# Placing row numbers and gates in bf16, and one block for a route and its expert layer

## The chip, the cores and the metric

The kernel runs on one core of one Trainium2 chip. The time is the device time of one execution in microseconds; what is compared is the median of several runs. Besides there is a profile of one execution.

## The reference

An attention layer with decaying state, then two mixture-of-experts layers, all over 3072 rows of 384 numbers (4 sequences of 768 steps, 8 heads of 48).

```
cur = u*k_t (x) v_t;  y_t = r_t (state + cur);  state = w*state + k_t (x) v_t
layer 1: rows with x.w_skip > 0:  e = argmax(x w_gate), g = softmax(x w_gate)[e]
         out = x + g * relu(x w1[e]) w2[e];  other rows: out = x
layer 2: the same for all rows, without the added x:  out = g * relu(x w1b[e]) w2b[e]
```

There are 8 experts of 384 x 1024 and 1024 x 384. Each row goes to one of them.

## The kernel before

`network` runs `attention`, then twice `route` and `moe`. The order on each engine is written out by hand, with semaphores between engines; `attention`, each `route` and each `moe` is a block of its own (`nc.Block()`), and at the end of a block every engine drains and waits for the others.

`route` makes a table. The 3072 rows lie as 24 tiles of 128: row r of tile i on partition r. For each row the route finds its expert, its rank among that expert's rows, and from them a place (`slot_i`) in a list in which each expert's rows begin at a tile of their own. The table has 128 partitions and NCOL columns (38 in the first layer, 45 in the second); column c holds the places of tile c: word 0 is the number of the row of x that stands there, word 1 its gate. Places that stay empty hold a number beyond the rows (NOWHERE), which the gathers skip.

Rows are put in their places by products. For tile i, `row_hot[:, i, :]` (128 x 128) is one where the row's place modulo 128 is the column, and `placing` (128 x 2 x NCOL) holds at the column of the row's place the row number and the gate. Their product, summed over the 24 tiles in one bank (`ps_placed`), is the table. All is f32. VectorE makes the column one-hots (L687), the gates' words (L690) and the row one-hots (L541, 8 of 3 tiles each); ScalarE makes the row numbers' words (L632, 24 small ones); TensorE multiplies (L617, which the profile shows as 48 records) after it has been kept busy by `stay_warm` (L22, 64 transposes of the identity). VectorE then writes `starts` (the spans of tiles of each expert) and the table (L709, L710).

Between these, ScalarE and VectorE split the first expert's weights in two fp32r parts (L763 `W.hi`: rounded; L768 `W.lo`: the residue). There are 6 pieces of w1 and 8 of w2. In the first route three of VectorE's pieces come before the table.

`moe` begins with a head: GpSimd gathers the first X row tiles by the table (L1006; X is 2 in the first layer, 4 in the second); TensorE loads its spans into registers, turns the identity (L1096 and 24 turns by `stay_warm`), then turns each gathered tile (L1090); ScalarE rounds it (L1244), VectorE takes the residue (L1314). Then comes a loop over the experts and, within one, over units of 192 or 256 rows (first layer) or 384 or 448 (second). In a unit the products to the hidden numbers go in 8 groups of 9 (L1107 to L1109: hi x hi, hi x lo, lo x hi for each of 3 chunks) through 4 banks; from the fifth group on TensorE waits for VectorE's residue of the hidden numbers (L1354) four groups before. VectorE makes pieces of the next weights between. The products back (`ps_y`) are scaled by the gate (L1331) and scattered by GpSimd. SyncE loads the weights.

## Time and profile before

| | |
|---|---|
| median of 3 runs | 570.91 us (569.67 to 571.74) |
| the profiled execution | 574.45 us, of which the span is 572.7 us |
| attention | until 133.6 us |
| first route, table written | 133.6 to 151.0 us |
| first layer's head, first expert product | 151.0 to 159.9 us |
| second route, table written | 310.8 to 328.1 us |
| second layer's head, first expert product | 328.1 to 338.1 us |
| TensorE busy | 94% of the span |

The span is what the trace covers; the execution's own time has 1.8 us around it. Engines: PE is TensorE, PEld its weight loads, DVE VectorE, ACT ScalarE, POOL GpSimd, SP SyncE; PEq and so on are their sequencers. A line such as L617 is that of the kernel. PEclk is the granted share of TensorE's clock of 2.4 GHz, 0.5 being its lower level of 1.2 GHz.

### The profile page before, as it was taken

To read this page: it belongs to the slowest core of one execution; us is meant where nothing else is said; L and a number is where in the kernel's file an instruction comes from. 1 tells how busy PE (TensorE), PEld (TensorE's weight loads), DVE (VectorE), ACT (ScalarE), POOL (GpSimd) and SP (SyncE) were. 2 spreads that over 40 slices of the span, in tenths; PEclk is the share of its full clock that TensorE was granted. 3 is DMA by queue.
4 is the path that set the end of the run, shared out by engine and by line. 5 is a ranking of instruction groups with operands and counts; after the bars stand their busy time and mean duration, and the time that the engine had idled before them with its cause. 6 is when DMAs were issued, how large, how long until landed. Compare 5 with 4: busy or idle time off the path is not lost. (4 is left out here: it accounts for less than half of the span.)

```text
span 572.7 us, 16167 instructions
## 1 busy us (share of the span) xinstructions
PE 537.0 (94%) x5557; PEld 510.8 (89%) x5558; DVE 381.7 (67%) x839; ACT 264.4 (46%) x758; POOL 247.4 (43%) x357
## 2 busy tenths in 40 slices
PE   4899999997889999999988879999999999999994
PEld 4789998986889999999976869999999999999994
DVE  4788888876788878888845727473747464737331
ACT  0233333333567656777733326362736352627230
POOL 5887778752144554444412061322433323324241
PEclk9999999997899999999999989999999999999998
DMA  8788889858177876774568523444444544111101
GB/s 154 127 178 166 161 163 175 166 203 286 31 251 255 256 232 195 227 256 130 159 197 284 177 81 132 162 149 151 165 155 150 169 138 155 51 43 46 42 1 40
DMA packets 114130, 89.60 MB, mean 156 GB/s; under 512 B 80672, under 2 KB 104931, under 8 KB 114080
## 3 DMA queue, kind: packets, MB, share of 16 engines
q1 hardware_dynamic: 105744, 73.96, 45.8%
q0 software_dynamic: 7776, 14.82, 9.4%
q8 instruction: 26, 0.43, 0.3%
q10 hardware_dynamic: 560, 0.20, 0.2%
q14 instruction: 24, 0.20, 0.1%
HBM read 80.44 MB, written 13.27 MB: 164 GB/s over the span
## 5 line engine op out<-in xcount | busy, mean ns | idle before, releaser
L768 DVE TENSOR_TENSOR w_lo<-w_raw,w_hi 128x384 fp32r<-128x384 f32 (+1 forms) x224 | 129.9, 606 | 5.4 <-ACT w_hi L763 3.4
L1107 PE MATMUL e_ps_h<-e_x_hi,w_hi 128*128 128x192 f32 (+3 forms) x384 | 119.9, 312 | 2.7 <-DVE e_x_lo L1314 2.7
L763 ACT CAST w_hi<-w_raw 128x384 fp32r<-128x384 f32 (+1 forms) x224 | 120.1, 566 | 4.4 <-issue 4.4
L1109 PE MATMUL e_ps_h<-e_x_hi,w_lo 128*128 128x192 f32 (+3 forms) x384 | 119.7, 312 | 0.5 <-issue 0.5
L1108 PE MATMUL e_ps_h<-e_x_lo,w_hi 128*128 128x192 f32 (+3 forms) x384 | 119.8, 312 | 0.0
L1354 DVE SCALAR_TENSOR_TENSOR e_h_lo<-e_ps_h,e_h_hi 128x128 fp32r<-128x128 f32 (+1 forms) x192 | 70.3, 395 | 45.2 <-ACT e_h_hi L1262 41.1
L1107 PE MATMUL e_ps_y<-w_hi,e_h_hi 128*128 128x384 f32 x272 | 95.6, 351 | 0.0
L1109 PE MATMUL e_ps_y<-w_hi,e_h_lo 128*128 128x384 f32 x272 | 91.4, 336 | 0.0
L1108 PE MATMUL e_ps_y<-w_lo,e_h_hi 128*128 128x384 f32 x272 | 91.3, 336 | 0.0
L1107 PEld LDWEIGHTS e_ps_h<-e_x_hi,w_hi 128*128 128x128 f32 x384 | 73.2, 191 | 5.1 <-DVE e_x_lo L1314 3.2
L1109 PEld LDWEIGHTS e_ps_h<-e_x_hi,w_lo 128*128 128x128 f32 x384 | 73.1, 190 | 0.9
L1108 PEld LDWEIGHTS e_ps_h<-e_x_lo,w_hi 128*128 128x128 f32 x384 | 73.1, 190 | 0.9
L1261 ACT ACTIVATE e_h_lo<-e_ps_h 128x64 fp32r<-128x64 f32 x128 | 29.2, 228 | 76.8 <-PE e_ps_h L1109 69.2
L1262 ACT ACTIVATE e_h_hi<-e_ps_h 128x256 fp32r<-128x256 f32 (+1 forms) x128 | 59.6, 465 | 0.0
L1314 DVE TENSOR_TENSOR e_x_lo<-e_ps_x,e_x_hi 128x384 fp32r<-128x384 f32 (+1 forms) x54 | 28.1, 523 | 43.9 <-ACT e_x_hi L1244 37.5
L1108 PEld LDWEIGHTS e_ps_y<-w_lo,e_h_hi 128*128 128x128 f32 x272 | 51.3, 188 | 0.0
L1107 PEld LDWEIGHTS e_ps_y<-w_hi,e_h_hi 128*128 128x128 f32 x272 | 51.2, 188 | 0.0
L1109 PEld LDWEIGHTS e_ps_y<-w_hi,e_h_lo 128*128 128x128 f32 x272 | 51.1, 188 | 0.0
L1244 ACT CAST e_x_hi<-e_ps_x 128x384 fp32r<-128x384 f32 (+1 forms) x54 | 24.4, 455 | 54.5 <-PE e_ps_x L1090 54.5
L1015 POOL DMA_INDIRECT x_in<-x_rows,e_ent_in x33 | 37.1, 1125 | 26.8 <-POOL e_ent_in L1011 22.0
L1027 POOL DMA_INDIRECT out_dram<-y_rows,e_ent_out x19 | 18.5, 974 | 62.5 <-DVE y_rows L1331 54.3
L224 ACT COPY xT<-ps_x 128x384 f32<-128x384 f32 x24 | 11.5, 480 | 71.0 <-PE ps_x L368 71.0
(192 smaller groups left out, 928.8 us busy)
## 6 DMA issues: line engine op xcount, KB each, us to landing
w_raw<-in_moe_w_dram SPq DMA_DIRECT2D x32, 1536.0 KB
r_in<-in_r_dram SPq DMA_DIRECT2D x24, 192.0 KB, 3.1
k_in<-in_k_dram SPq DMA_DIRECT2D x24, 192.0 KB, 3.9
v_in<-in_v_dram SPq DMA_DIRECT2D x24, 192.0 KB, 3.9
x_rows<-rows SPq DMA_DIRECT2D x24, 192.0 KB, 3.5
w_raw<-x_rows SPq DMA_DIRECT2D x4, 768.0 KB, 7.8
e_late_x<-x_rows SPq DMA_DIRECT2D x2, 768.0 KB, 6.1
x_in<-x_rows,e_ent_in POOLq DMA_INDIRECT x33, 3.0
```

What stands on the lines that cost most here:

```text
L763: act.copy(self._of(self.hi1[par], self.hi2[par], n), self._of(self.raw1[par], self.raw2[par], n)).then_inc(self.hi_done[par], 1)
L768: eng.tensor_tensor(self._of(self.lo1[par], self.lo2[par], n), self._of(self.raw1[par], self.raw2[par], n), self._of(self.hi1[par], self.h ...
L1015: pool.indirect_dma_start(x_in[n][:], None, rows, bass.IndirectOffsetOnAxis(ap=ent_in[n][:, 0:1], axis=0), bounds_check=bound, oob_is_err= ...
L1027: pool.indirect_dma_start(out_rows, bass.IndirectOffsetOnAxis(ap=ent_out[slot][0:count, 0:1], axis=0), y_rows[slot][0:count, :], None, bou ...
L1107: pe.matmul(o, s_hi, m_hi, start=(k == 0), stop=False)
L1108: pe.matmul(o, s_hi, m_lo, start=False, stop=False)
L1109: return pe.matmul(o, s_lo, m_hi, start=False, stop=(k == last))
L1244: act.copy(x_hi[:, :, w], ps_x[n % 2][:, 0:D].rearrange("p (c t) -> p c t", c=DC)[:, :, 0:w.stop - w.start]).then_inc(x_hi_done, 1)
L1261: act.activation(h_lo[:, k, top_at:top_at + HALF], ps_h[k % 4][:, TOP], ACT.Relu).then_inc(h_top_done, 1)
L1262: act.activation(h_hi[:, k, :], ps_h[k % 4][:, 0:XW], ACT.Relu).then_inc(h_hi_done, 1)
L1314: dve.tensor_tensor(x_lo[:, :, w], ps_x[n % 2][:, 0:D].rearrange("p (c t) -> p c t", c=DC)[:, :, 0:w.stop - w.start], x_hi[:, :, w].bitcas ...
L1354: ins = dve.scalar_tensor_tensor(h_lo[:, k, lo_at[n]:lo_at[n] + of.stop - of.start], ps_h[k % 4][:, of], 0.0, h_hi[:, k, of].bitcast(F32), ...
```

## The change

1. A route and its layer are in one block. In place of the block's end, semaphores (`routed`, `gates_split`, `gates_placed`) hold back what needs the table.
2. Layouts are turned: `row_hot` is [128, 128 columns, 24 tiles] and `col_is` [128, NCOL, 24], with the tile as the inner dimension, in bf16. They come from 16-bit integers: `at` (row and column of each place) and one large `iota` [128, 128, 24] that GpSimd makes once. The column one-hots are one instruction, the row one-hots three (8 tiles each).
3. The row number is placed as two bf16 words that are added afterwards: `tile_word` (128 x the tile's number, less NOWHERE, which is now 4096; VectorE multiplies) and `own_word` (the partition; ScalarE multiplies). A first product of `ones` and `empty` adds NOWHERE to every place. The products read `row_hot[:, :, i]` and `id_words[:, :, :, i]`.
4. Gates leave the route. GpSimd splits them in three bf16 pieces; VectorE spreads these over the columns right behind the table (two instructions), and TensorE places them in the layer's head, 12 tiles before the first gathered tile is turned and 12 after it, into `ps_y[1]`; VectorE adds the three and writes word 1 of the table. `stay_warm` there has 1 turn of 8 in place of 3.
5. VectorE's first pieces of w1 go from the route to the head: all 6 before the first `x_low`, all 8 of w2 after the gates.
6. GpSimd copies only word 0 of the table for its gathers and scatters. The layer's tiles stand in another order in memory.

```
-            for n in range(PLACES):
-                if n % (PLACES // 2) == 0:
-                    pe.wait_ge(gates_placed, 2 * n // PLACES + 1)
-                pe.wait_ge(ids_placed, n + 1)
+            pe.wait_ge(words_made, 4)
+            pe.matmul(ps_ids, ones[:], empty[:], start=True, stop=False)
+            pe.wait_ge(tile_words, 1)
+            pe.wait_ge(own_words, 1)
+            for n, part in enumerate(PARTS):
                 pe.wait_ge(rows_ready, n + 1)
-                for q in range(GP):
-                    i = GP * n + q
-                    ins = pe.matmul(ps_placed, row_hot[:, i, :], placing[:, 2 * NCOL * i:2 * NCOL * (i + 1)], start=(i == 0), stop=(i == TILES - 1))
-                ins.then_inc(placed, 1)
+                for i in range(part.start, part.stop):
+                    ins = pe.matmul(ps_ids, row_hot[:, :, i], id_words[:, :, :, i], start=False, stop=(i == TILES - 1))
+            ins.then_inc(placed, 1)
...
-            for place in range(PLACES):
-                if place % (PLACES // 2) == 0:
-                    act.wait_ge(col_equal, 2 * place // PLACES + 1)
-                for i in range(GP * place, GP * place + GP):
-                    ins = act.mul(col_hot[:, i, 0, :], col_is[:, i, :], entry[:, i, 0:1])
-                ins.then_inc(ids_placed, 1)
+            act.mul(id_words[:, 1, :, :].rearrange("p c i -> p (c i)"), col_is[:].rearrange("p c i -> p (c i)"), own_word[:, 0:1]).then_inc(own_words, 1)
...
-            for n in range(2):
-                i = slice(TILES // 2 * n, TILES // 2 * (n + 1))
-                wide = [P, TILES // 2, NCOL]
-                dve.tensor_tensor(col_is[:, i, :], row_iota[:, 0:NCOL].unsqueeze(1).to_broadcast(wide),
-                                  col_i[:, i].unsqueeze(2).to_broadcast(wide), ALU.is_equal).then_inc(col_equal, 1)
-                dve.wait_ge(col_equal, n + 1)
-                dve.tensor_tensor(col_hot[:, i, 1, :], col_is[:, i, :], entry[:, i, 1].unsqueeze(2).to_broadcast(wide), ALU.mult).then_inc(gates_placed, 1)
-                for place in range(PLACES // 2 * n, PLACES // 2 * (n + 1)):
-                    rows_hot(dve, place)
-            if m == 0:
-                for n in range(W.N1 // 2):
-                    W.lo(dve, 0, 0, n)
+            dve.tensor_tensor(col_is[:], iota[:, 0:NCOL, :], at[:, 1, :].unsqueeze(1).to_broadcast([P, NCOL, TILES]), ALU.is_equal).then_inc(col_equal, 1)
+            link(dve.tensor_scalar(at[:, 0, :], slot_i[:], P - 1, None, ALU.bitwise_and))
+            dve.tensor_tensor(id_words[:, 0, :, :], col_is[:], tile_word[:].unsqueeze(1).to_broadcast([P, NCOL, TILES]), ALU.mult).then_inc(tile_words, 1)
+            for part in PARTS:
+                dve.tensor_tensor(row_hot[:, :, part], iota[:, :, part], at[:, 0, part].unsqueeze(1).to_broadcast([P, P, part.stop - part.start]), ALU.is_equal).then_inc(rows_ready, 1)
...
-            dve.wait_ge(placed, PLACES)
-            dve.tensor_scalar(table[:, 0:NCOL, 0], ps_table[:, 0, :], float(NOWHERE), None, ALU.add)
-            dve.tensor_copy(table[:, 0:NCOL, 1].bitcast(F32), ps_table[:, 1, :])
+            dve.wait_ge(placed, 1)
+            link(dve.tensor_reduce(ids[:], ps_ids.rearrange("p w c -> p c w"), AX.X, ALU.add))
+            dve.tensor_copy(table[:, 0:NCOL, 0], ids[:]).then_inc(routed, 1)
...
+            pe.wait_ge(routed, 1)
             start_spans(pe)
...
-            stay_warm(pe, ident, ps_y[0][:, 0:P], 3)
-            for n in range(X):
+            stay_warm(pe, ident, ps_y[0][:, 0:P], 1)
+            for n, some in enumerate(HALVES):
+                pe.wait_ge(gates_spread, n + 1)
+                for i in range(some.start, some.stop):
+                    ins = pe.matmul(ps_gates, row_hot[:, :, i], gate_words[:, :, :, i], start=(i == 0), stop=(i == TILES - 1))
+                if n == 0:
+                    turn_x(0, 0)
+            ins.then_inc(gates_placed, 1)
+            for n in range(1, X):
                 turn_x(0, n)
...
-            dve.sem_inc(y_done, 1)
+            dve.wait_ge(gates_split, 5)
+            for some in HALVES:
+                wide = [P, 3, NCOL, some.stop - some.start]
+                dve.tensor_tensor(gate_words[:, :, :, some], col_is[:, :, some].unsqueeze(1).to_broadcast(wide), pieces[:, :, some].unsqueeze(2).to_broadcast(wide), ALU.mult).then_inc(gates_spread, 1)
+            dve.wait_ge(routed, 1)
             start_spans(dve)
...
             if m == 0:
-                for n in range(W.N1 // 2, W.N1 + 2):
+                for n in range(W.N1):
                     W.lo(dve, 0, 0, n)
             for n in range(X):
                 x_low(0, n)
-            if m == 0:
-                for n in range(W.N1 + 2, W.N):
+            dve.wait_ge(gates_placed, 1)
+            dve.tensor_reduce(table[:, 0:NCOL, 1].bitcast(F32), ps_gates.rearrange("p w c -> p c w"), AX.X, ALU.add).then_inc(y_done, 1)
+            if m == 0:
+                for n in range(W.N1, W.N):
                     W.lo(dve, 0, 0, n)
...
+            with ExitStack() as both:
+                block = both.enter_context(nc.Block())
+                late = route(nc, both, block, m, W, ...)
+                moe(nc, both, block, m, W, ..., *late)
```

## Rows read from the trace of the kernel before

**Rows 1.** The page: TensorE's line, and its clock by slice.

```profile
PE 537.0 (94%) x5557; PEld 510.8 (89%) x5558; DVE 381.7 (67%) x839; ACT 264.4 (46%) x758; POOL 247.4 (43%) x357
...
PEclk9999999997899999999999989999999999999998
```

**Rows 2.** Timeline, first route: start, us taken, engine, line, operation.

```profile
136.66 8.65 PE L22 MATMUL m_ps_spare<-ident 128*128 128x128 f32 x64
...
141.64 0.63 DVE L687 TENSOR_TENSOR m_col_is<-m_row_iota,m_col_i 128x456 f32<-128x456 int32 x1
...
142.86 1.96 DVE L541 TENSOR_TENSOR m_row_hot<-m_row_iota,m_row_i 128x384 f32<-128x384 int32 x4
...
145.15 5.48 PE L617 MATMUL m_ps_places<-m_placing,m_row_hot 128*128 128x76 f32 x48
...
148.02 3.39 ACT L763 CAST w_hi<-w_raw 128x384 fp32r<-128x384 f32 x8
...
150.78 0.19 DVE L710 COPY table<-m_ps_places 128x38 f32<-128x38 f32 x1
```

**Rows 3.** Timeline, head of the first layer and first expert.

```profile
152.63 1.21 POOL L1006 DMA_INDIRECT rows<-x_rows,table  x1 [15.83 <-issue]
...
152.88 0.63 PE L1096 MATMUL e_ps_h<-ident 128*128 128x128 f32 x4 [2.24 <-issue]
...
153.34 4.45 PE L22 MATMUL e_ps_y<-ident 128*128 128x128 f32 x24
...
154.14 1.54 POOL L1006 DMA_INDIRECT x_in<-x_rows,table  x1 [0.30 <-issue]
...
157.96 0.49 PE L1090 MATMUL e_ps_x<-ident,x_in 128*128 128x128 f32 x3
...
159.60 2.91 DVE L768 TENSOR_TENSOR w_lo<-w_raw,w_hi 128x384 fp32r<-128x384 f32 x6
...
159.94 0.35 PE L1107 MATMUL e_ps_h<-e_x_hi,w_hi 128*128 128x192 f32 x1 [1.50 <-DVE e_x_lo L1314]
...
161.03 0.28 PE L1107 MATMUL e_ps_h<-e_x_hi,w_hi 128*128 128x192 f32 x1
...
162.44 0.48 DVE L1354 SCALAR_TENSOR_TENSOR e_h_lo<-e_ps_h,e_h_hi 128x128 fp32r<-128x128 f32 x2
```

**Rows 4.** Timeline, second route and head of its layer.

```profile
313.20 0.50 PE L606 MATMUL m_ps_places<-m_chosen,m_ones 128*128 128x192 bf16 x1 [1.13 <-DVE m_chosen L659]
313.52 0.27 PE L607 MATMUL m_ps_places<-m_chosen,m_neg_lower 128*128 128x192 bf16 x1
...
322.28 5.49 PE L617 MATMUL m_ps_places<-m_placing,m_row_hot 128*128 128x90 f32 x48
...
327.93 0.20 DVE L710 COPY table<-m_ps_places 128x45 f32<-128x45 f32 x1
...
329.26 1.10 POOL L1006 DMA_INDIRECT rows<-x_rows,table  x1 [12.99 <-issue]
...
333.28 1.00 POOL L1006 DMA_INDIRECT x_in<-x_rows,table  x1 [0.30 <-issue]
...
336.36 0.55 PE L1090 MATMUL e_ps_x<-ident,x_in 128*128 128x128 f32 x3 [0.79 <-DMA x_in<-x_rows,table]
...
338.14 0.68 PE L1107 MATMUL e_ps_h<-e_x_hi,w_hi 128*128 128x384 f32 x1 [1.24 <-DVE e_x_lo L1314]
```

**Rows 5.** Lines 606, 607: ns min/median/max, first and last start, shapes.

```profile
L606 PE MATMUL m_ps_places<-m_chosen,m_ones x2: 500/502/503, 136.2 to 313.2; 128*128 128x192 bf16 x2
...
L607 PE MATMUL m_ps_places<-m_chosen,m_neg_lower x2: 266/302/337, 136.5 to 313.5; 128*128 128x192 bf16 x2
```

**Rows 6.** Line 677, the same columns.

```profile
L677 DVE TENSOR_TENSOR m_pos<-m_ps_places,m_seen x2: 612/614/617, 139.2 to 316.3; 128x192 f32<-128x192 f32 x2
```

**Rows 7.** Line 1002, GpSimd's first instruction in the layer's block.

```profile
L1002 POOLq MOVE  x2: 29/29/29, 151.6 to 328.4; - x2
```

**Rows 8.** Window 338 to 342 us; chain of waits there.

```profile
338.00:342.00 4.00, 3.86 (x14) 3.86 (x15) 0.00 (x0) 0.63 (x3) 2.47 (x4) 0.61 0.22 60
...
338.83 0.32 PE e_ps_h L1108
...
341.50 0.17 PE e_ps_h L1108
```

## What I expect of the change

> **What bounds the kernel now.** I read the page first: TensorE is busy 94% of the span [rows 1], so time can be won or lost only where TensorE does work that is not the expert products, or waits. The slices of the page show where: its granted clock dips between 129 and 157 us and again from 329 us (tenth, eleventh and 24th slice of 14.3 us) [rows 1]; together with the names of the lines this leads to two places, the two routes with the head of the expert layer behind each. I then read the timeline of each, since a share of busy time hides order there.
>
> Route of the first layer [rows 2]: TensorE turns the identity 64 times until 145.31 us, only to keep warm. VectorE starts the column one-hots at 141.64 us, and the placing products run from 145.15 to 150.63 us: 48 records in 5.48 us, 0.114 us each, 24 products of two passes. So TensorE sets the end here, as the first product starts when the warming ends. The table is written by 150.97 us. The route of the second layer has the same form: 5.49 us of placing from 322.28 us, the table at 328.13 us [rows 4].
>
> Head of the first layer [rows 3]: GpSimd's first gather starts at 152.63 us, 1.66 us behind the table; the second row tile is turned at 157.96 us and the first expert product starts at 159.94 us, 8.97 us behind the table. Between them lie 4.45 us of warming, which end at 157.79 us. Head of the second: table 328.13, first gather 329.26, fourth gather 333.28, its turn 336.36 (3.08 us later), first product 338.14 us: 10.01 us [rows 4]. The gathers, 1.34 us apart, set that one.
>
> **What the change does with each, in a sum.** Times are given behind the table (R) where that is shorter.
>
> *The row numbers.* The 24 products in f32 (48 records) become 24 in bf16 plus one short one that fills in the empty places. Both operands are now read with a step: tiles are the inner dimension of the one-hots and of the words, so neighbouring weight columns and neighbouring moving columns are 24 elements, 48 bytes, apart. No row shows that exactly. The nearest is the product of L606, whose moving operand is read 16 bytes apart: 0.50 us for 192 columns in both instances, beside 0.27 to 0.34 us for L607, whose operand has no step [rows 5]. Some 0.08 us of the 0.50 is that it comes first after a wait and 0.19 us is what every record carries beyond its columns (L607 at full clock: 0.27 less 192 columns at 2.4 GHz, 0.08). That leaves about 0.24 us, 1.25 ns a column, where the operand without step has 0.42. Taken whole, 0.32 us from L606's start to L607's [rows 4] is 1.67 ns. VectorE's L677, which reads 96 bytes apart, has 0.61 us for 192 elements, where 384 without a step take 0.55 [rows 2, 6]; less some 0.13 us fixed that is 2.5 ns an element, the worst row there is. The weights have 128 columns, more than the 76 or 90 that move, and weight loads overlap with products (in the first expert 192 columns take no longer than the load: 0.11 us a product), so the pace is that of the load: 0.06 to 0.10 us if the step costs the load nothing (0.10 is the record of a bf16 load), 128 x 1.25 = 0.16, 128 x 1.67 = 0.21, or 128 x 2.5 = 0.32 us. I take 0.16, from the nearest row, and keep both ends. 24 x 0.16 plus 0.1 for the short product is 3.95 us, so the products end at 149.1 in place of 150.63, and at 326.2 in place of 327.77: **-1.5 and -1.55 us**.
>
> VectorE must be ahead of that. It makes 912 + 912 + 3 x 1024 elements in five instructions where it made 4 x 456 + 8 x 384 in twelve: the same 4896. By the four of L541 in 1.96 us, 0.47 us for 384 [rows 2], an instruction costs 1.04 ns an element and 0.07 us. From 141.45 us that makes the three parts of the row one-hots ready at about 144.95, 146.1 and 147.3 us; TensorE wants them at 145.15, 146.5 and 147.8. Nothing is late, even if the 16-bit types bring no speed at all. ScalarE's word of 912 elements replaces 24 small products and lies under VectorE. GpSimd's large iota (3072 elements) comes before 139 us, and its five small instructions that split the gates wait for nothing that is wanted soon. Hidden, all of it: VectorE first needs them behind the table.
>
> *The table.* One reduction and a copy that waits for it replace two independent copies. By L710 (0.19 us) that is 0.5 us against 0.34: **+0.15 us, twice, +0.3**.
>
> *The block between route and layer.* All engines now go on at a semaphore. In the first layer the block ended at 151.6 us, when ScalarE was done with its 8 casts at 151.41 [rows 2, 7]; in the second at 328.4 [rows 7], 0.25 us behind the table. GpSimd then still needs about 1.0 us before its first gather (151.6 to 152.63). So the gather starts at R + 1.1 in both, against 1.66 and 1.13: 0.5 us in the first layer and nothing in the second. Whether it counts depends on TensorE.
>
> *The gates, now in the head.* 2 x 12 products stand in TensorE's queue between the warming (8 turns in place of 24) and the turns of the row tiles. TensorE: register loads until R + 1.1 (152.88 less 151.6, and the semaphore), 12 turns of the identity until 2.5. The moving operand has 114 and 135 columns; the pace by the same rate is 0.16 and 0.17 us. First layer: first half until 4.4, tile 0 (landed at 1.1 + 3.1 = 4.2) until 4.85, second half until 6.8, then tile 1 (landed at 5.7), and from there 1.98 us to the first product as before (157.96 to 159.94): 8.8 against 8.97, **-0.2 us**. Second layer: halves end at 4.55 and 7.05, tiles 1 and 2 by 7.95; tile 3 waits until the residue of tile 1 is taken out of its bank, 8.8 (its gather landed at 8.2); plus 1.78 us to the product: 10.55 against 10.01, **+0.5 us**. VectorE: two gate products of 1.5 us each at one element a cycle, then six residues of w1 at 0.6 us (three stood in the route before, under TensorE's products), free at 6.7, before tile 1's cast at about 7.4. Hidden.
>
> *Behind the head of the first layer.* VectorE had 6 residues of w2 left before the first hidden residue, from 159.60 us to 162.44, and that one was done 3.0 us after the first product [rows 3]; now it has the reduction of the gates (about 0.3 us) and 8, so it comes some 1.3 us later. TensorE wants it for its fifth group; a group of nine products takes 1.09 us at first (159.94 to 161.03 us) [rows 3] and 1.0 after, so 4.0 us after its start; it will come at some 4.4: **+0.45 us**, and VectorE has no slack to give it back for the rest of this product.
>
> *The clock.* In the second head TensorE is nearly idle from the end of the warming to 338.14 us, and the granted clock of 338 to 342 is 0.61 [rows 8]: the first ten or so products take 0.32 us where they take 0.17 a little later, 1.5 us lost. With the gates' products there it is busy until R + 7 and idle for stretches under a microsecond after that. I expect full clock at the first product: **-1.5 us**.
>
> The sum is -1.5 - 1.55 + 0.3 - 0.2 + 0.5 + 0.45 - 1.5 = **-3.5 us**. The profiled execution, 574.45 us with 572.7 of span, would have 571; it is 3.5 above the median of the runs shown, 570.91, so the median goes to **567.4 us**. A measurement here tells 0.3% (1.7 us) from nothing.
>
> On the operands' step the Trainium skill (Advanced Engine Details and Errata, Memory Cachelines) speaks against the change: accesses that each hit another 16-byte line of SBUF pay a penalty. L606 agrees as far as a row can [rows 5]. It gives no price; with the penalty of L606 on both operands my sum is what stands above, without it -5 us.
>
> **Rivals.** *The step costs TensorE nothing on loads and little on columns* (pace 0.10 or less). Then VectorE sets the routes: 147.3 + 0.8 = 148.1 (-2.6) and 325.5 (-2.2), the head of the first layer is set by VectorE's queue (free at 6.7, two residues, product at 8.0: -1.0), the second stays at the gathers (0), with +0.3 and +0.45: -5.05 us; if VectorE is twice as fast on 16-bit operands, up to -6.5: **564.4 to 565.9 us**. For it: all records of weight loads in the trace have no step, so only the moving side is shown to pay. Chance 0.27. The Trainium skill (VectorE: DVE Perf Modes, The perf-mode tier table) has `tensor_tensor` at 2x when all is 16-bit; no row shows it, and it counts only in this case, for the last 1.4 us.
>
> *The load with a step is dear.* Place: the 24 weight loads of each of the four placements. Each 0.01 us more on the pace costs 24 x 0.01 x 4 = 0.96 us. The gain is gone at a pace of 0.196 us, and it is slower by over 0.3% from 0.214, which is L606's upper reading. At 0.213: -3.5 + 5.1 = +1.6, **572.5 us**; at VectorE's 2.5 ns, +11.9, **582.8 us**. Loads that do not overlap (0.16 + 0.10) come to the same side. For it: 48 bytes are further apart than L606's 16, and both operands step at once. Against it: L606's moving operand paid only 1.25 ns. Chance 0.20.
>
> *Nothing measurable*: pace 0.18 to 0.21, or 0.16 with the clock still falling in the second head (+1.5) and at half in the first as well (there it is full at 159.94 because of the long warming that is cut; another 1.5): -0.5 us, **569.2 to 572.6 us**. Chance 0.15. The forecast itself, pace 0.12 to 0.18, has 0.38, with its own range of 565.5 to 569.2.
>
> So faster 0.65, same 0.15, slower 0.20. The range goes from 563.8 (the fast end, a little more) to 573.2, which leaves out most of the dear loads.
>
> **What would show it.** In the trace after: the interval of the row-number products in both routes (0.16 us; 0.10 or 0.21 decide the rivals); the row one-hots 1.2 us each, or 0.6; R to the first gather 1.1 us; the first expert product at R + 8.8 and R + 10.5; its interval in the second layer 0.17 us at once; a wait of about 0.4 us on VectorE before the fifth group of the first expert. The prediction is wrong if the interval is not near 0.16, if the gates end later than tile 1's landing by more than I have, or if fetching the code after the removed block end costs time that the trace does not show now.

## The result, and the profile after

The change makes the kernel slower. Its median is 575.93 us (575.41 to 577.75, 4 runs), that of the kernel before 570.5 us on the same chip (569.67 to 571.74, 4 runs): a ratio of 1.0099, interval 1.0068 to 1.013. I had predicted 567.4 us, and the value lies above my range. The profiled execution took 577.75 us, with a span of 576.0; before it was 574.45 and 572.7.

The page's clock by slice shows the two places again. Both dips are longer than before [rows 1], and the second reaches a 5.

```profile
PE 543.3 (94%) x5527; PEld 512.8 (89%) x5528; DVE 381.3 (66%) x831; ACT 255.9 (44%) x712; POOL 255.5 (44%) x372
...
PEclk9999999997789999999998859999999999999998
```

The timeline of the first route and head of the changed kernel (start, us taken, engine, line, operation) is to be read against [rows 2, 3]:

```profile
134.00 3.12 POOL L576 IOTA iota<- 128x3072 int16 x1
...
135.30 1.86 DVE L665 TENSOR_SCALAR m_den<-m_den 128x24 f32<-128x24 f32 x1
...
141.59 0.63 DVE L687 TENSOR_TENSOR m_col_is<-iota,m_at 128x912 bf16<-128x912 int16 x1
...
143.74 3.54 PE L623 MATMUL m_ps_ids<-m_id_words,m_row_hot 128*128 128x76 bf16 x24 [0.78 <-DVE m_row_hot L693]
...
147.66 0.19 DVE L709 CAST table<-m_ids 128x38 int32<-128x38 f32 x1
...
148.14 1.56 POOL L1014 DMA_INDIRECT rows<-x_rows,table  x1 [8.01 <-DVE table L709]
...
148.97 1.08 PE L1105 MATMUL e_ps_h<-ident 128*128 128x128 f32 x4 [1.69 <-issue]
...
151.55 2.63 PE L1110 MATMUL e_ps_y<-m_gate_words,m_row_hot 128*128 128x114 bf16 x12
...
154.35 2.61 PE L1110 MATMUL e_ps_y<-m_gate_words,m_row_hot 128*128 128x114 bf16 x12
...
158.76 0.53 PE L1123 MATMUL e_ps_h<-e_x_hi,w_hi 128*128 128x192 f32 x1 [1.16 <-DVE e_x_lo L1335]
...
322.64 4.09 PE L623 MATMUL m_ps_ids<-m_id_words,m_row_hot 128*128 128x90 bf16 x24
...
327.12 0.19 DVE L709 CAST table<-m_ids 128x45 int32<-128x45 f32 x1
...
330.84 3.08 PE L1110 MATMUL e_ps_y<-m_gate_words,m_row_hot 128*128 128x135 bf16 x12
...
341.18 0.68 PE L1123 MATMUL e_ps_h<-e_x_hi,w_hi 128*128 128x384 f32 x1 [0.99 <-DVE e_x_lo L1335]
```

The placing of row numbers takes 3.54 and 4.09 us in place of 5.48 and 5.49, so the routes gain. The gates' halves take 2.6 and 3.1 us each, and the first expert product comes 10.91 us behind the table (158.76 less 147.85) and 13.87 us behind it (341.18 less 327.31), where it was 8.97 and 10.01. Busy time and granted clock in windows of 3 us show in what state TensorE went through the two heads. The last three columns are the clock, the DMA share and GB/s; the first of the pairs before them is TensorE's busy time.

```profile
core 0: us, PE busy (x) PEld busy (x) DVE busy (x) ACT busy (x) POOL busy (x), PEclk, DMA share, GB/s
150.00:153.00 3.00, 3.00 (x17) 2.58 (x16) 3.00 (x5) 0.00 (x0) 1.50 (x1) 0.50 0.36 96
153.00:156.00 3.00, 3.00 (x18) 2.31 (x17) 0.56 (x2) 0.48 (x1) 0.61 (x2) 0.96 0.38 84
156.00:159.00 3.00, 1.84 (x9) 1.27 (x8) 0.85 (x3) 0.48 (x1) 1.14 (x3) 0.60 1.03 422
159.00:162.00 3.00, 3.00 (x15) 3.00 (x16) 3.00 (x7) 0.97 (x3) 2.11 (x3) 0.50 0.34 118
...
330.00:333.00 3.00, 3.00 (x14) 2.15 (x14) 0.00 (x0) 0.00 (x0) 2.39 (x3) 0.50 0.53 149
333.00:336.00 3.00, 3.00 (x14) 2.14 (x13) 0.56 (x1) 0.48 (x1) 0.33 (x2) 0.50 0.28 92
336.00:339.00 3.00, 2.70 (x12) 1.85 (x10) 0.39 (x1) 0.74 (x2) 0.00 (x0) 0.50 0.00 0
```

The second head runs at 0.50, the level of 1.2 GHz, from 330 us to its first product, although TensorE is busy for 3.00 of 3.00 us in two of these windows. The first head is at 0.50 to 0.60 but for the window from 153 us, and the first expert products behind it are at 0.50.

The difference of the two spans, piece by piece (VectorE's first instruction of a route, the table, the first expert product as marks):

| stretch | before | after | difference | in my sum |
|---|---|---|---|---|
| attention, until 133.65 / 132.28 | | | -1.37 | 0 |
| first route until the table | 17.32 | 15.57 | -1.75 | -1.35 |
| table to first product | 8.97 | 10.91 | +1.94 | -0.2 |
| first product to second route | 150.93 | 152.76 | +1.83 | +0.45 |
| second route until the table | 17.26 | 15.79 | -1.47 | -1.4 |
| table to first product | 10.01 | 13.87 | +3.86 | +0.5 |
| the rest | 234.56 | 234.82 | +0.26 | -1.5 |

They add up to +3.3 us. Nothing in the change touches attention: its end lies between 131.79 and 133.65 us in the profiles of this study, so that row is scatter of single executions, and what the change itself did is +4.7 us, near the 5.4 us between the medians.

Each profile is one execution, and one wait in them comes and goes: near the end of the first layer TensorE waits 1.4 to 1.7 us (L1216 here, L1200 before) in 6 of the 18 profiles, these two among them, and not in the others. It lies in the stretch from first product to second route, so where two kernels are compared by that stretch, it is said which of them has the wait.

### The profile page after: what moved, and what is told of

It reads as the page before. It is cut to its first block and busy times, and to the rows that moved or that the text cites. A ratio compares the mean times of both kernels' runs of the same rounds, so it can differ in the third digit from the quotient of the medians.

```text
span 576.0 us, 16027 instructions
## 1 busy us (share of the span) xinstructions
PE 543.3 (94%) x5527; PEld 512.8 (89%) x5528; DVE 381.3 (66%) x831; ACT 255.9 (44%) x712; POOL 255.5 (44%) x372
```

## The experiments

Every kernel below also bounds the loop counts that it reads from the table of spans from below by zero (`max` with 0 on the register behind each load). The first run is the changed kernel with only that. Each was compared with the kernel before on its own chip; a ratio under 1 is faster than before. Where there was a single run, the two numbers stand without an interval.

| run | median us (runs) | ratio to before, interval |
|---|---|---|
| changed kernel, bounded | 576.43 (4) | 1.0115 [1.0063, 1.0168] |
| gates without step | 568.73 (10) | 0.9953 [0.9927, 0.998] |
| only the moving operand without step | 566.35 (1) | before 571.95 |
| only the weights without step | 578.2 (1) | before 571.95 |
| gates left out | 567.94 (9) | 0.9948 [0.9922, 0.9974] |
| 24 turns, stepped | 582.75 (4) | 1.0195 [1.0151, 1.0239] |
| 24 turns, moving operand without step | 571.68 (1) | before 571.32 |
| iota early | 575.87 (10) | 1.0075 [1.0047, 1.0104] |
| tiles outside | 569.62 (10) | 0.9957 [0.9926, 0.9988] |
| words outside, written with a step | 593.47 (5) | 1.0384 [1.0367, 1.04] |
| the same, iota early | 592.51 (5) | 1.0382 [1.0359, 1.0405] |
| the same, turns behind the row numbers | 592.64 (5) | 1.0371 [1.0352, 1.0389] |
| tiles outside, turns behind the row numbers | 571.96 (12) | 0.9996 [0.9975, 1.0017] |
| mixed layout | 566.84 (6) | 0.9911 [0.9883, 0.9939] |
| mixed, late turns too | 566.1 (7) | 0.991 [0.9871, 0.9949] |
| mixed, late turns only | 564.79 (6) | 0.9883 [0.9857, 0.991] |

**The changed kernel, bounded.** 

> The changed kernel with one addition that all kernels of these experiments have: a register that is loaded with a span is taken as the larger of it and 0, some 0.03 us at each load. All theories: 575 to 578 us, 1% above before; the granted clock at half from 147 us to 154 and again from 157 to 164, and from 327 to 344 us.

 It shows what the changed kernel shows (clock 0.962, VectorE held for 1.86 us, 11.42 us from table to first product), so the bounds do not disturb the comparison. One thing differs: from 153 to 156 us the clock was 0.50 here and 0.96 in the changed kernel. So a rise of the clock in a single profile is not a fixed property of the code.

**The gates' operands without a step.**

```
-ins = pe.matmul(ps_gates, row_hot[:, :, i], gate_words[:, :, :, i], ...)
+ins = pe.matmul(ps_y[1][:, 0:3 * NCOL], row_hot[:].rearrange("p c i -> p (c i)")[:, P * i:P * i + P],
+                gate_words[:].rearrange("p w c i -> p (w c i)")[:, 3 * NCOL * i:3 * NCOL * i + 3 * NCOL], ...)
```

> The gates' 24 products in each head read other, neighbouring elements of the same two tiles (weights and moving operand both without a step), so the gates are not those of the reference; number and size of the products stay. Theory A (the step is what costs: 1.9 ns a moving column, and TensorE so fed counts as little active, so the clock falls): 12 products take 1.3 us or less in place of 2.6 and 3.1, the clock recovers before the first expert product in both layers, 569 to 572 us. Theory B (the clock falls because TensorE idles about 1 us behind the row numbers and the warming was cut to a third): products shorter, but the clock stays low until after the start of the expert products, 573 to 575 us. Theory C (neither: the block or the moved residues cost): no change, 576 us.

 Twelve products took 1.34 and 1.02 us in the first layer. The kernel was 7.7 us faster than the bounded one, and faster than before. So the step of these 48 products, with what follows from it, is more than the whole loss. The wrong gates do not change the amount of work (5527 products in both profiles). The clock was not full throughout: 0.55 from 159 to 162 us and 0.54 from 333 to 336 us, under the first expert products of both layers.

**One operand at a time**, as above but for one of the two.

> Gates' products again, the weights stepped as in the change, only the moving operand read without a step (other elements, so the gates are not the reference's). If the moving operand is what pays, as the pace so far says (1.9 ns times 76, 90, 114 and 135 columns, and never the 128 of the weights): 0.06 to 0.12 us a product and 568 to 570 us as without any step. If the weights pay as well (rival of the forecast): 0.16 to 0.21 us a product and 572 us or more.

> The mirror of that: weights without a step (other elements, so the gates are not the reference's), the moving operand stepped. If the moving operand pays: 0.22 and 0.26 us a product, the clock at half as in the change, 575 to 577 us. If the weights pay: 0.12 us or less, 569 us.

Weights with the step, moving operand without:

```profile
152.80 1.35 PE L1117 MATMUL e_ps_y<-m_gate_words,m_row_hot 128*128 128x114 bf16 x12
154.59 1.35 PE L1117 MATMUL e_ps_y<-m_gate_words,m_row_hot 128*128 128x114 bf16 x12
```

Weights without the step, moving operand with it:

```profile
152.66 2.59 PE L1117 MATMUL e_ps_y<-m_gate_words,m_row_hot 128*128 128x114 bf16 x12
155.68 2.59 PE L1117 MATMUL e_ps_y<-m_gate_words,m_row_hot 128*128 128x114 bf16 x12
```

Both at a clock of about half. There the moving operand pays everything and the weights nothing that shows: 566.35 beside 578.2 us, each a single run and each some 1 to 2 us beyond what was forecast for it. At full clock the weights' step does show, as the mixed layout below tells.

**The gates left out**, with 24 turns of the identity as before the change (in outline).

```
-dve.tensor_tensor(gate_words[...], ...)    -pe.matmul(ps_gates, ...) x24    -dve.tensor_reduce(table[:, 0:NCOL, 1], ps_gates, ...)
+dve.memset(table[:, 0:NCOL, 1].bitcast(F32), 0.5)
-stay_warm(pe, ident, ps_y[0][:, 0:P], 1)
+stay_warm(pe, ident, ps_y[0][:, 0:P], 3)
```

> Leaves the gates' spreading, products and reduction out (every gate is 0.5) and has 3 warming turns in the head again; row numbers stay as in the change. Theories A and B: the heads are as before, the routes keep their gain of 1.75 and 1.5 us: 567 to 569.5 us, 0.3 to 0.6% under before. Theory C (the shared block or VectorE's moved residues cost time in the head or first unit): 572 us or more.

 567.94 us: without gates, the shared block, the row numbers and the moved residues together are a gain of 0.5%. Gates placed without a step (568.73, with 8 turns) cost nothing that can be told from that.

**The change with 24 turns**, and **the same with the gates' moving operand without its step**.

```
-stay_warm(pe, ident, ps_y[0][:, 0:P], 1)
+stay_warm(pe, ident, ps_y[0][:, 0:P], 3)
```

> The change with 3 turns of warming in the head in place of 1; gates as in the change. Theory A: the added 16 turns go in front of the gates at half clock, 0.21 us each, 3.4 us in each head, and do not keep the clock up through the stepped products: 578 to 583 us. Theory B: the clock is up at the first expert product in both layers, which gives back 1.5 to 3 us a layer against the 16 turns: 572 to 576 us.

> The run with 3 turns of warming in the head again, and the gates' moving operand without a step (other elements, so the gates are not the reference's); the weights stepped. The only difference from that run (582.75 us) is the step of the moving operand. Theory A (TensorE fed with a stepped moving operand loses its clock, however busy its row in the profile): the clock that the 24 turns bring back is kept, 1.0 at the first expert product of both layers, 568 to 571 us. Theory A' (the step costs only its own time, the clock falls for other reasons): 24 products save some 2.5 us in the first layer and 3 in the second, 576 to 578 us, the clock falls behind the first expert product as it did.

Windows of the first head, stepped:

```profile
153.00:156.00 3.00, 3.00 (x16) 3.00 (x15) 0.91 (x2) 0.00 (x0) 0.00 (x0) 0.50 0.31 56
156.00:159.00 3.00, 3.00 (x18) 2.31 (x17) 0.00 (x0) 0.00 (x0) 0.00 (x0) 0.99 0.97 358
159.00:162.00 3.00, 3.00 (x16) 2.11 (x13) 0.56 (x1) 0.48 (x1) 1.22 (x2) 0.58 0.43 158
162.00:165.00 3.00, 1.84 (x9) 1.75 (x9) 2.36 (x6) 0.48 (x1) 1.41 (x3) 0.50 0.21 63
165.00:168.00 3.00, 3.00 (x16) 3.00 (x16) 3.00 (x8) 1.50 (x5) 2.27 (x2) 0.50 0.08 23
```

The same stretch, moving operand without step, and the end of the second head:

```profile
153.00:156.00 3.00, 3.00 (x26) 3.00 (x25) 0.76 (x2) 0.00 (x0) 0.00 (x0) 0.74 0.41 66
156.00:159.00 3.00, 1.84 (x23) 1.60 (x21) 1.25 (x4) 0.96 (x2) 1.41 (x3) 1.00 0.92 378
159.00:162.00 3.00, 3.00 (x27) 3.00 (x28) 3.00 (x8) 1.50 (x5) 1.75 (x2) 1.00 0.59 186
162.00:165.00 3.00, 2.94 (x26) 2.77 (x26) 3.00 (x10) 2.89 (x10) 2.27 (x2) 1.00 0.30 66
...
336.00:339.00 3.00, 3.00 (x11) 3.00 (x10) 0.48 (x1) 1.17 (x3) 1.92 (x4) 0.52 0.02 3
```

This pair is the heart of the study. Besides the step, the second kernel only lets the first half of the gates wait for all the words, which are there at 150.15 us, 5 us before TensorE turns to them. In the first kernel the turns bring the clock to 0.99; then the stepped products keep TensorE "busy" for 3.00 of 3.00 us, and the clock falls to 0.58 and stays at half for some 10 us. In the second TensorE is busy for only 1.84 of 3.00 us in the same place and keeps its clock. So the busy time of the records does not tell which of the two keeps it. The stepped halves take 2.61 us at a clock of 0.99, as much at 0.58 just behind, and 2.63 at 0.50 in the changed kernel: their pace is that of the reading, not of the clock.

The second head limits this. Without the step the clock held through the gates there (1.00 from 330 to 333 us), but fell to 0.52 under the first expert products, so the clock was full at the first product of both layers, as the theory wanted, but held behind it in the first only. And the gates with the step also last longer, about 6 us in a head in place of 2: whether it is the way of reading or the longer stretch of small work that brings the clock down was not tested.

Between the two medians lie 11 us (on two chips; against before on its own chip, 12.6 and 0.4 us). Between the two profiled executions it is 12.5 us: 7.4 are the four halves themselves (11.3 us in place of 4.0), 4.4 the stretch from first product to second route (153.29 against 148.89), of which 1.4 is the wait that only the stepped one has. So most of the difference is the products' own time, and the clock behind them is some 3 us, all of it in the first layer.

**The large iota at the end of attention** (`pool.iota` moved from the route, behind attention's last GpSimd work).

> The changed kernel with GpSimd's iota of 3072 elements at the end of the attention block, where GpSimd idles, in place of in the route. VectorE's L665 of 24 elements took 1.86 us there and ended with that iota. Theory D (the iota holds VectorE up over a port that both use): L665 takes 0.27 us again, the row one-hots are ready 1.6 us earlier, TensorE then starts at the end of its warming, 0.5 to 0.8 us earlier: 0.5 to 0.8 us under the bounded control, 575.7 us. Rival: L665 stays slow, no gain.

 VectorE's instruction of 24 elements, held for 1.86 us beside the iota, took 0.30 us here, and the row numbers were placed about 0.4 us earlier. The time (1.0075) cannot be told from that of the changed kernel (1.0099).

**Tiles as the outer dimension everywhere** (in outline).

```
-row_hot [P, P, TILES]   col_is [P, NCOL, TILES]   gate_words [P, 3, NCOL, TILES]   id_words [P, 2, NCOL, TILES]   iota [P, P, TILES]
+row_hot [P, TILES, P]   col_is [P, TILES, NCOL]   gate_words [P, TILES, 3, NCOL]   id_words [P, TILES, 2, NCOL]   iota [P, P]
+four parts of 6 tiles; all one-hots broadcast the place over the columns
```

> The change with its tensors turned back: the tile is the outer dimension of the one-hots and words, all bf16, so neither operand of TensorE has a step in routes or heads; the iota has 128 elements; VectorE's broadcast operand has an innermost step of 0 (4 parts of 6 tiles). Theory A: products at 0.06 to 0.10 us; VectorE at one element a cycle (912 in 1.1 us, 768 in 0.87 us) sets the routes; table 2.5 to 3 us after the start of the placing, heads at the gathers; the clock stays up: 564 to 567 us, about 1% under before. Rival (VectorE's halved pace costs what TensorE gains): 568 to 570 us, as without a step in the gates alone.

 The six products of a part take 0.37 to 0.39 us and wait 0.3 to 0.5 us for VectorE, which is slower now: 1.11 us for 912 elements in place of 0.63. The table still comes at 147.4 us, the gates take 1.34 and 1.13 us, and the kernel is 0.4% faster than before, as the rival had it.

**Words outside, one-hots inside.** The words are written by VectorE and ScalarE with a step, so that TensorE reads them without one; then with the early iota, then with 16 turns behind the row numbers.

```
+id_words [P, TILES, 2, NCOL], gate_words [P, TILES, 3, NCOL]
+dve.tensor_tensor(id_words[:, :, 0, :].rearrange("p i c -> p c i"), col_is[:], ...)
+act.mul(id_words[:, :, 1, :].rearrange("p i c -> p c i"), col_is[:], ...)
```

> The change with only the words (row numbers and gates, the moving operands) laid out with the tile outside; the one-hots of the rows, the weights, keep their step and VectorE its two elements a cycle for them. Row products at 0.06 to 0.10 us, ready when VectorE is; VectorE's three writes of words now go with a step (912, 1368 or 1620 elements), 1.1 us or up to 2.1 for 912. The table 1 to 1.5 us earlier than with all tiles outside; the iota still holds VectorE up: 565.5 to 568 us. Rival (VectorE pays for writing with a step, 2 ns an element): 568 to 570 us.

> The same with the iota at the end of the attention block. In the first route TensorE and VectorE are then ready at about the same time: 0 to 1.5 us under the one before.

> The same with 16 turns of the identity behind the row numbers' products, while VectorE writes the table and TensorE would idle. If the clock falls in the head because TensorE idles there: it stays at 1.0 until the gates, the head's 12 turns take 1.4 us in place of 2.6, and the first expert products of the second layer no longer run at half: 1 to 3 us less. Rival: it only delays TensorE's register loads, nothing or 0.3 us more.

The first missed by some 26 us, and the other two, which were forecast from it, by as much. The timeline of the first:

```profile
142.32 4.26 ACT L635 ACTIVATE m_id_words<-m_col_is,m_own_word 128x912 bf16<-128x912 bf16 x1 [5.77 <-DVE m_col_is L687]
142.35 4.15 DVE L691 TENSOR_TENSOR m_id_words<-m_col_is,m_tile_word 128x912 bf16<-128x912 bf16 x1
...
147.16 1.89 PE L623 MATMUL m_ps_ids<-m_id_words,m_row_hot 128*128 128x76 bf16 x24 [3.63 <-DVE m_row_hot L693]
...
149.55 12.40 DVE L1334 TENSOR_TENSOR m_gate_words<-m_col_is,m_gate_pieces 128x1368 bf16<-128x1368 bf16 x2
149.93 6.46 POOL L1021 DMA_INDIRECT rows<-x_rows,table  x1 [9.79 <-DVE table L709]
```

A write of single bf16 elements with a step costs 4.15 us for 912, 4.5 ns each, on VectorE and on ScalarE alike (the two ran side by side; neither was tried alone), where I had allowed 1 to 2 ns. The gates' words take 6.2 us each in place of 0.82. GpSimd's gather beside them takes 6.46 us in place of 1.56. TensorE's part behaved as hoped (24 products in 1.89 us), but it was not the price. Against this one the early iota (592.51 us, forecast 0 to 1.5 us less) and the turns behind the row numbers (592.64 us) change nothing that can be told from noise, though with the turns the clock was 1.00 from 147 to 153 us, where it was 0.50 with the early iota alone.

**Turns behind the row numbers**, added to the kernel with tiles outside.

```
 ins.then_inc(placed, 1)
+stay_warm(pe, ident, ps_spare[:], 2)
```

> The version with the tile as the outer dimension everywhere (569.62 us), and 16 turns of the identity more behind the row-number products. What it asks: is the clock's fall at the beginning of the head the work of TensorE's idle time behind those products? There it stood at 0.50 from 147 to 153 us after 2.3 us without work. Theory: yes. Then the turns end some 0.3 us before the registers are loaded, the granted clock of 147 to 153 is near 1.0, the head's 12 turns take 1.4 us in place of 2.6, and the first product comes about 1 us earlier in the first layer; the second layer, which the gathers set, gains nothing: 568.5 us. Rival: the clock falls whatever TensorE does there, or the head is set by VectorE's gate words (3.07 us behind the table) and the gathers: 569.6 us, and the first product stays at 8.3 us behind the table.

```profile
150.00:153.00 3.00, 1.98 (x24) 1.80 (x23) 3.00 (x4) 0.00 (x0) 2.09 (x2) 1.00 0.21 66
153.00:156.00 3.00, 1.67 (x18) 1.30 (x18) 3.00 (x7) 0.96 (x2) 1.38 (x2) 1.00 0.13 32
156.00:159.00 3.00, 2.28 (x11) 2.29 (x11) 3.00 (x9) 0.01 (x1) 2.19 (x4) 0.57 0.88 259
159.00:162.00 3.00, 3.00 (x16) 3.00 (x16) 2.47 (x8) 1.70 (x6) 2.00 (x3) 0.50 0.99 367
```

The windows show the first half of the theory right: the clock is 1.00 through the head, and the turns there take 1.04 us in place of 1.91. But the gain is given back: the clock falls just behind, under the first expert products, which are full work. From first product to second route it is 153.56 us, where it was 150.59 without the turns (both have the wait, of 1.7 and 1.4 us). The median is 0.9996 of before, where the kernel without the turns had 0.9957; the two intervals just overlap, so the profiles show the loss and the medians only suggest it.

**The mixed layout.** Row one-hots as in the change (tile inside; VectorE writes without a step, at two elements a cycle; TensorE reads them as weights with a step), the words with tiles outside, the large iota at the end of attention, the 16 turns kept.

```
+row_hot [P, P, TILES]   (read row_hot[:, :, i] as weights)
+id_words [P, TILES, 2, NCOL]   gate_words [P, TILES, 3, NCOL]   col_is [P, TILES, NCOL]
```

> As the one before, but with the row one-hots as in the change: tile inside, read by TensorE as weights with a step (which cost nothing where the gates were tried), in three parts of 1024 elements at two elements a cycle; the words of row numbers and gates stay with the tile outside. The large table of column numbers is made at the end of attention. If stepped weights are free here as well, VectorE's 3.45 us for the row one-hots becomes 1.89 us, in both routes, the products behind the last part take under 1 us, and the tables are written 1.5 us earlier each: 3 us below the one before, 565.5 us. Rival: the weights' step costs at this pace (0.06 us a product, where the gates' products had 0.11), so the products take 0.1 us or more each, and nothing is gained: 568.5 us.

 24 products took 1.83 us in the first route, 0.076 each, with the weights 48 bytes apart. That is far below the 0.147 with a stepped moving operand, but not free. The gates' halves at full clock show it, stepped weights first (114 and 135 columns), then without any step (tiles outside, with the turns):

```profile
149.72 0.98 PE L1119 MATMUL e_ps_y<-m_gate_words,m_row_hot 128*128 128x114 bf16 x12
321.33 0.99 PE L1119 MATMUL e_ps_y<-m_gate_words,m_row_hot 128*128 128x135 bf16 x12
...
151.19 0.79 PE L1118 MATMUL e_ps_y<-m_gate_words,m_row_hot 128*128 128x114 bf16 x12
328.80 0.90 PE L1118 MATMUL e_ps_y<-m_gate_words,m_row_hot 128*128 128x135 bf16 x12
```

With the step on the weights the time does not grow with the columns. From the start of one product to that of the next it is 0.070 us at 76 as at 135 columns; without any step it is 0.036 and 0.062 us. So here the pace is that of the load, and for the row numbers it is about double. In the gates' kernels at half clock the columns took longer than that, which hid it.

From the route's start to the table it is 14.1 us, against 15.57 in the changed kernel. The clock still fell behind the head:

```profile
153.00:156.00 3.00, 1.44 (x14) 1.20 (x12) 3.00 (x8) 0.48 (x1) 1.49 (x3) 1.00 0.43 51
156.00:159.00 3.00, 3.00 (x18) 3.00 (x17) 3.00 (x9) 1.61 (x6) 2.01 (x3) 0.56 0.99 401
...
330.00:333.00 3.00, 3.00 (x11) 3.00 (x12) 0.00 (x0) 0.28 (x2) 1.48 (x3) 0.57 0.02 3
```

**Turns in the last wait of the head**, with and without those behind the row numbers.

```
             for n in range(1, X):
                 turn_x(0, n)
+            stay_warm(pe, ident, ps_y[0][:, 0:P], 1)
```

> The mixed layout (566.84 us) with 8 turns of the identity more in each head, behind the turns of the last row tile, where TensorE waited 1.56 and 1.29 us for VectorE's residue. There the granted clock was still 1.00 and fell just behind: to half from 156.3 to 159.6 us and from 330.3 to 333.5 us, under the first expert products. Theory: the clock answers to the short waits in the last microseconds of the head, as it did to the stepped gates; with 0.9 us of turns in the last wait it stays at 1.00, and the first products of both layers gain half of 3.2 us each: 3.2 us, 563.6 us. Rival: the clock falls by the waits between the row tiles too, and comes down as before: 566.8 us.

> As the one before, but without the 16 turns behind the row-number products. Theory: those turns only keep the clock up where VectorE's gate words and the gathers set the pace; the head's 12 turns take 2.6 us in place of 1.4, still before the gate words are there or little after, and the first product comes at most 0.5 us later; what counts is the clock at the first product: within 0.5 us of the one before, 563.6 to 564.1 us. Rival: the late turns can't hold what has fallen before, the clock is at half again under the first products: 567 us.

Windows of the kernel with late turns only:

```profile
150.00:153.00 3.00, 2.82 (x28) 2.55 (x27) 3.00 (x6) 0.48 (x1) 1.08 (x2) 0.62 0.35 97
153.00:156.00 3.00, 2.00 (x19) 1.77 (x18) 2.79 (x7) 0.48 (x1) 1.55 (x3) 1.00 0.39 90
156.00:159.00 3.00, 3.00 (x29) 3.00 (x29) 3.00 (x9) 1.94 (x6) 2.11 (x3) 1.00 1.03 419
...
330.00:333.00 3.00, 3.00 (x19) 3.00 (x18) 1.28 (x3) 1.83 (x5) 1.58 (x4) 1.00 0.02 3
```

Full clock at the first product of both layers, and 148.5 us from there to the second route, against 150.28 in the mixed layout without the late turns (none of the three has the wait). With both sets of turns the first layer was the same (148.6 us), while in the second head the clock fell to 0.70 and 0.74 between 324 and 330 us. Its runs spread from 562.88 to 569.63 us, so the two medians cannot be told apart. The last kernel, 564.79 us, is the fastest of the study and 1.2% faster than the one before.

What the late turns are worth in time is not settled by this. Added to the mixed layout and nothing else changed, they left the median where it was (0.991 of before against 0.9911; 563.6 us was forecast, and three of seven runs were near it). The kernel with late turns only has 0.9883, and its interval overlaps both. The mixed layout without any added turns was not run. The gain of the mixed layout over before is clear in all three; that of the late turns is seen in the profiles' clock alone.

## Why the prediction was wrong

**What bounds the kernel, and where the change acts:** right. But for attention's scatter, all differences lie in the two routes, the two heads and what the clock does behind them.

**The row numbers:** the size was right (-1.35 and -1.4 with the table's tail; -1.75 and -1.47 measured), the reason wrong. I wrote that "the pace is that of the load". The paces are 0.147 us at 76 columns, 0.170 at 90, 0.218 at 114 and 0.256 at 135: they grow with the columns that move, by some 1.85 ns each ((0.256 - 0.147) / 59), and with unstepped weights they stay (2.59 us for 12, in place of 2.6). The stepped load has a pace of its own, 0.070 us, which lies under these. My 0.16 us (128 x 1.25 ns) lay near 76 x 1.85 = 0.14 and 90 x 1.85 = 0.17 by chance. The rival "the load with a step is dear" fell for the same reason: it had the right sign, and its 0.21 us and 572.5 us were the nearest in size, but it had the wrong operand.

**The gates in the head:** here the sum failed. "The moving operand has 114 and 135 columns; the pace by the same rate is 0.16 and 0.17 us": with the rate put to the right operand, and by the upper reading of L606 that I had beside it (1.67 ns a column), it would have been 0.19 and 0.23. Measured are 0.218 and 0.256. That is 48 products x about 0.07 us = 3.4 us, in the way of the row tiles' turns.

**The clock:** the other failed step, and the larger: "I expect full clock at the first product: -1.5 us". I took busy for warm. The second head was at half clock from 330 us on and the first for most of its length: the 12 turns took 2.6 us where I had 1.4; the clock was 0.50 from 159 to 162 us, where before the products had full speed; the first expert products of the second layer took 0.32 us until 344.2 as before. By the table, the two heads and what stands behind them missed the sum by 8.6 us; 3.4 are the gates' pace, and the other 5 or so, by subtraction, go with the clock. "At half in the first as well" stood in my rival "nothing measurable", for want of the long warming. But the long warming alone does not bring it back: with it the kernel takes 582.75 us, since the 32 added turns take about 6 us themselves and the clock falls during the stepped gates behind them.

Two causes of the low clock can be told apart. That the head starts at half is not the step's work: the kernel with tiles outside, which has no step, takes the same 1.08 + 1.91 us for its 12 turns, and 16 turns in TensorE's wait behind the row numbers make that 0.63 + 1.04. That the clock does not come back, or falls again before the first product, goes with the stepped moving operand: in the pair with 24 turns it fell during the gates with the step, in both heads, and held through them without it (with the caution above on their length). What happens just behind the first product is a third thing, and the step does not decide it: without any step the clock fell there in some profiles (0.55, 0.54, 0.57) and held in others.

**The block removed:** the gather came 0.3 us behind the table in place of my 1.1, TensorE's first turn 1.1 us behind it, as I had it. In the first layer it was worth nothing, since TensorE set the end.

**Behind the head:** I forecast a wait of about 0.4 us for VectorE before the fifth group. VectorE's first hidden residue came 3.8 us behind the first product, but TensorE at half clock got there later still; the wait did not appear. The 1.83 us lost there go with the clock, at 0.50 from 159 to 162 us (both profiles have the late wait, so it drops out).

**VectorE hidden, iota hidden:** not in the first route. The warming took 7.52 us in place of 8.65, and TensorE then waited 0.78 us for VectorE's row one-hots (L693). The instructions themselves were fast enough: 16-bit operands in step 1 ran at two elements a cycle (912 in 0.63 us), as the Trainium skill has it (VectorE: DVE Perf Modes, What auto-detection actually checks); where the place is broadcast over the inner dimension, with step 0, it is one (1.11 us), which agrees too. It was the iota that was not hidden: it held VectorE for 1.6 us. With the iota early the table came 0.46 us sooner behind the route's start (15.09 against 15.55 us), so it cost about half a microsecond.

**A slip in my rival:** the total of "the step costs TensorE nothing on loads", -5.05 us, leaves out the clock's -1.5 us that the forecast has, and gives no reason; with it the rival would have stood near 564.4 us. It changes nothing here.

**What I weighed wrong:** the Trainium skill's page on cachelines (Advanced Engine Details and Errata, Memory Cachelines) was a warning in the right direction, though it names neither a price nor the operand that pays. Read with L606 [rows 5], it could have made the gates, with 1.5 times the columns of the row numbers, the dear part. I priced the step by an operand without asking which of the two had paid in the only row that showed it; it was the moving one.

**Open:** why the clock falls some microseconds behind a stretch in which TensorE had waits but was often busy (the mixed layout: 1.00 until 156 us, then 0.56), why the same code shows it in one profile and not in another, and what in the stepped products it answers to. The Trainium skill (TensorE: Matmul & The Clock Gate, HAM oscillation — how this bites in real kernels) has waits between bursts bring the clock down, so that the next burst starts cold. The mixed layout goes that way, with 0.56 in the three microseconds behind a window with 1.44 us of work; the stepped kernel with 24 turns fell while its records show no wait at all, which that rule does not cover.

## What to carry to other kernels

Lay out operands so that what moves through TensorE has no step; if a step must be somewhere, put it on the weights, where it cost up to 0.034 us a product here and not 0.1 to 0.2, and not on the write of 2-byte elements (4.5 ns each). A price read from a row belongs to the operand that paid it: scale it by that operand's columns. A stretch of small work ahead of the main products is paid twice, once itself and once in the clock that those products start with; look at the granted clock there and not at the busy time. Turns in the last wait before them kept it at 1.00 in the profiles; that this wins time the medians here do not show.

## What was unexpected of the hardware

- A moving bf16 operand with elements 48 bytes apart costs 1.85 ns a column at either clock (for 12 x 114 columns 2.61 us at 0.99 and 2.63 at 0.50). As weights the same step costs nothing that shows at half clock (1.35 us for 12, where 1.34 without), and at full clock it sets a pace of 0.070 us a product, whatever the columns (0.98 and 0.99 us for 12, where 0.79 and 0.90 without).
- TensorE loses its clock in such products while its records show it busy: 0.99 to 0.58 between two windows that both have 3.00 us of work.
- Writing 912 bf16 elements with a step takes 4.15 us on VectorE and 4.26 us on ScalarE, side by side (0.63 and 1.05 without), and a gather on GpSimd beside such a write 6.46 us in place of 1.56.
- A GpSimd iota of 3072 16-bit elements (3.12 us) held a VectorE instruction of 24 elements for 1.86 us in place of 0.27.
- Warming early can move the loss: 16 turns that kept the clock at 1.00 through the head were followed by its fall under the first expert products (0.57 and 0.50 from 156 to 162 us), which ran at 1.00 in the kernel without them.
